# Attention, channel mixing and an eight-expert MoE on one core: who makes the experts' low weight parts, and where the routing steps stand in the queues

## The reference, cut to what matters

```python
logits = x @ w_gate                       # 8 experts
local_gate = sigmoid(x @ w_local)
for s in range(S):                        # per batch row
    fresh_e = argmax(logits[b, s])
    e = fresh_e if s == 0 or local_gate[b, s] < 0.5 else prev_e
    prev_e = e
    p = softmax(logits[b, s])
    h = maximum(x[b, s] @ w1[e], 0)       # 512 -> 1024
    out[b, s] = p[e] * (h @ w2[e])        # 1024 -> 512
```

## Time and profile before

| | us |
|---|---|
| median of 3 runs | 630.22 (628.58 to 631.71) |
| the profiled execution, whole time | 632.64 |
| its span in the trace | 630.8 |
| TensorE busy | 611.1 (97% of the span) |
| VectorE busy | 421.8 (67%) |
| ScalarE busy | 321.1 (51%) |
| GpSimd busy | 176.6 (28%) |

### The profile page before, as it was taken

How to read it: one execution, slowest core, us unless ns; L and a number is a source line. 1 busy time by engine, 2 the same in 40 slices (tenths; PEclk the granted TensorE clock), 3 DMA queues, 4 the chain that set the end, 5 groups by cost and what they waited for, 6 DMA issues and landing times.

```text
span 630.8 us, 14748 instructions
## 1 busy us (share of the span) xinstructions
PE 611.1 (97%) x4474; PEld 506.3 (80%) x4475; DVE 421.8 (67%) x1167; ACT 321.1 (51%) x698; POOL 176.6 (28%) x261
## 2 busy tenths in 40 slices
PE   8989999999999999999999899689999999999996
PEld 6878888888888888889889777568878888878885
DVE  4767779755788797686889958863772633683541
ACT  5766779687426605713527553343851612662531
POOL 4545445600000000000000600535572351184141
PEclk9999999999999999999999999979999999999999
DMA  8987886002200010010024552477792441385000
GB/s 312 372 264 244 275 276 200 18 4 81 100 35 0 1 68 0 0 47 22 0 96 179 177 217 68 131 233 236 226 330 92 156 174 48 118 308 212 20 17 15
DMA packets 32935, 84.66 MB, mean 134 GB/s; under 512 B 4602, under 2 KB 7418, under 8 KB 32896
## 3 DMA queue, kind: packets, MB, share of 16 engines
q1 hardware_dynamic: 26816, 70.03, 32.4%
q0 software_dynamic: 3200, 8.92, 4.1%
q10 hardware_dynamic: 2880, 5.24, 2.5%
HBM read 76.04 MB, written 9.70 MB: 136 GB/s over the span
## 4 chain that ended last, share of the span: by engine, by line
PE 94%; DVE 2%; issue 2%; ACT 1%; POOL 0%; DVEq 0%; ACTq 0%; POOLq 0%
PE banks L891 24%; PE banks L893 23%; PE banks L892 23%; PE banks L762 4%; PE banks L829 3%; PE banks L1081 3%; PE banks L838 2%; PE banks L792 2%; PE banks L776 2%; PE banks L806 1%; PE banks L802 1%; PE banks L1000 1%; PE banks L853 1%; DVE we_lo L1535 1%; DVE table L1755 1%
## 5 line engine op out<-in xcount | busy, mean ns | idle before, releaser
L1502 DVE CUSTOM_DVE_ANT_0 product<-x,xT 128x512 f32<-128x512 f32 x120 | 77.6, 686 | 1.4 <-DMA xT<-in_w 1.4
L891 PE MATMUL banks<-we_hi,xg_hi 128*128 (+1 forms) x160 | 66.2, 413 | 9.9 <-DVE we_lo L1535 8.0
L1799 ACT ACTIVATE prob<-neg,negmax 128x160 f32<-128x160 f32 (+1 forms) x136 | 59.1, 436 | 30.5 <-DVE negmax L1210 20.8
L1777 DVE TENSOR_SCALAR hid<-banks 128x512 f32<-128x512 f32 x34 | 23.5, 691 | 72.0 <-PE banks L893 70.8
L891 PE MATMUL banks<-we_hi,hid_hi 128*128 (+1 forms) x160 | 67.2, 420 | 0.3 <-DVE hid_lo L1616 0.2
L1909 ACT ACTIVATE k_sum<-banks 128x512 f32<-128x512 f32 (+2 forms) x40 | 21.4, 534 | 88.4 <-PE banks L893 84.8
L651 POOL TENSOR_TENSOR we_lo<-raw_end,we_hi 128x512 f32 (+1 forms) x36 | 54.6, 1545 | 35.4 <-ACT we_hi L1889 35.3
L893 PE MATMUL banks<-we_hi,xg_lo 128*128 (+1 forms) x160 | 63.8, 399 | 0.0
L892 PE MATMUL banks<-we_lo,xg_hi 128*128 (+1 forms) x160 | 63.6, 398 | 0.0
L893 PE MATMUL banks<-we_hi,hid_lo 128*128 (+1 forms) x160 | 62.7, 392 | 0.0
L892 PE MATMUL banks<-we_lo,hid_hi 128*128 (+1 forms) x160 | 62.6, 391 | 0.0
(11 more groups left out here) (298 smaller groups left out, 1465.9 us busy)
## 6 DMA issues: line engine op xcount, KB each, us to landing
xT<-in_w_e SPq DMA_DIRECT2D x36, 512.0 KB, 4.5
raw_end<-in_w_e SPq DMA_DIRECT2D x36, 512.0 KB, 5.3
qk<-in_qk_t SPq DMA_DIRECT2D x32, 448.0 KB, 6.3
vw<-in_v_t SPq DMA_DIRECT2D x32, 256.0 KB, 5.5
w_raw<-in_w_mix ACTq DMA_DIRECT2D x20, 256.0 KB, 4.3
x_rows<-x SPq DMA_DIRECT2D x17, 256.0 KB, 2.0
xT<-in_w SPq DMA_DIRECT2D x8, 256.0 KB, 3.6
vz<-in_v_z SPq DMA_DIRECT2D x8, 128.0 KB, 3.4
```

The costliest lines, as they stand in the source:

```text
L891: pe.matmul(dst, left[0], right[0], start=first, stop=False)
L1502: dve.tensor_tensor_reduce(product[:, k % 2, :], x2[:, t, :], w9(e), 1.0, 0.0, ALU.mult, ALU.add, dot[:, t % 2, e:e + 1]).then_inc(dotted, 1)
L1777: dve.tensor_scalar(hid[:, D * h:D * (h + 1)], ps_h[:, h, :], 0.0, None, ALU.max).then_inc(hid_ready, 1)
L1799: act.activation(prob[:, t % 2, c], neg[:, c], ACT.Exp, scale=-1.0, bias=negmax[:, t % 2, k:k + 1], accum_out=rsum[:, t % 2, k:k + 1]).the ...
```

## The change

GpSimd waits, before the first expert's parts 6 and 7, until VectorE has made all six of its own. For the second expert, GpSimd makes none: VectorE makes the parts 4 to 7 in a row, and GpSimd only waits for them before it scatters tile 2. The computation of `table` moves ahead of `rest_of_hidden(2, 0)`, behind the one-hot matrices of the gates. On VectorE `rest_of_hidden(0, 0)` now comes before `fresh_choice(final)` and `rest_of_hidden(0, 1)` before the logit differences and `runs`. On TensorE `turn_keeps`, `turn_last_runs` and `turn_carries` move one or two steps of `outputs(0)` later, and `turn_chosen` and `count_picks` move into `hidden(1)`, whose steps are `c`.

```diff
@@ GpSimd
             gather(2, 0, NA * P)
+            pool.wait_ge(we_lo_ready, VPARTS + VPARTS)
             last_parts(0, slice(0, 1))
@@ GpSimd, after scatter(0) and scatter(1)
-            last_parts(1, slice(1, 2))
+            pool.wait_ge(we_last_lo_ready, 3 * LPARTS)
             pool.wait_ge(y_stored[0], 16)
             scatter(2, 0)
@@ TensorE
             outputs(0, 0, first, range(0, 1))
-            turn_keeps(final)
             turn_hidden(0, 1)
             outputs(0, 0, first, range(1, 3))
+            turn_keeps(final)
+            outputs(0, 0, first, range(3, 5))
             turn_last_runs(final)
-            outputs(0, 0, first, range(3, 5))
+            outputs(0, 0, first, range(5, 7))
             turn_carries(final)
-            outputs(0, 0, first, range(5, 7))
-            turn_chosen(final)
             outputs(0, 0, first, range(7, FC)).then_inc(y_summed, 1)
...
             hidden(1, first, 0, range(0, 1))
+            turn_chosen(final)
+            hidden(1, first, 0, range(1, 3))
             count_picks(final)
-            hidden(1, first, 0, range(1, DC)).then_inc(hid_summed, 1)
+            hidden(1, first, 0, range(3, DC)).then_inc(hid_summed, 1)
@@ VectorE
+            rest_of_hidden(0, 0)
             fresh_choice(final)
-            rest_of_hidden(0, 0)
+            rest_of_hidden(0, 1)
             dve.tensor_tensor(ldiff[:], logit[:, :, 0:E], by_token(lmax[:], E), ALU.subtract).then_inc(diff_ready, 1)
             runs(final)
-            rest_of_hidden(0, 1)
             carries(final)
...
             ins.then_inc(gate_onehots_ready, 1)
-            rest_of_hidden(2, 0)
-            rest_of_part(1, slice(1, 2), 2)
-            dve.wait_ge(gates_summed, 1)
...
-            rest_of_part(1, slice(1, 2), 3)
-            rest_of_hidden(2, 1)
-            rest_of_rows(3)
+            end = ntile[0:1, 1, :].unsqueeze(1).broadcast_to([1, LATER, E])
...
+            dve.tensor_copy(table[:, MT + EARLY:2 * MT], differs).then_inc(tables_ready, 1)
+            rest_of_hidden(2, 0)
+            rest_of_part(1, slice(1, 2), 2)
+            dve.wait_ge(gates_summed, 1)
...
+            rest_of_part(1, slice(1, 2), 3)
+            rest_of_hidden(2, 1)
+            rest_of_rows(3)
-            for j in range(PARTS // 2, VPARTS):
+            for j in range(PARTS // 2, PARTS):
                 rest_of_part(1, slice(1, 2), j)
```

More of the change, by code:

```diff
@@ L1727, in _ @@
             ins.then_inc(gate_onehots_ready, 1)
-            rest_of_hidden(2, 0)
-            rest_of_part(1, slice(1, 2), 2)
-            dve.wait_ge(gates_summed, 1)
-            dve.tensor_reduce(slot_gate[:, 0:EARLY], ps_chain_odd[:, 0:3 * EARLY].rearrange("p (k m) -> p m k", k=3), AX.X, ALU.add)
-            dve.tensor_reduce(slot_gate[:, EARLY:MT], ps_chain[:, 0:3 * LATER].rearrange("p (k m) -> p m k", k=3), AX.X,
-                              ALU.add).then_inc(gates_ready, 1)
-            rest_of_part(1, slice(1, 2), 3)
-            rest_of_hidden(2, 1)
-            rest_of_rows(3)
             end = ntile[0:1, 1, :].unsqueeze(1).broadcast_to([1, LATER, E])
@@ L1755, in _ @@
             dve.tensor_copy(table[:, MT + EARLY:2 * MT], differs).then_inc(tables_ready, 1)
-            for j in range(PARTS // 2, VPARTS):
+            rest_of_hidden(2, 0)
+            rest_of_part(1, slice(1, 2), 2)
+            dve.wait_ge(gates_summed, 1)
+            dve.tensor_reduce(slot_gate[:, 0:EARLY], ps_chain_odd[:, 0:3 * EARLY].rearrange("p (k m) -> p m k", k=3), AX.X, ALU.add)
+            dve.tensor_reduce(slot_gate[:, EARLY:MT], ps_chain[:, 0:3 * LATER].rearrange("p (k m) -> p m k", k=3), AX.X,
+                              ALU.add).then_inc(gates_ready, 1)
+            rest_of_part(1, slice(1, 2), 3)
+            rest_of_hidden(2, 1)
+            rest_of_rows(3)
+            for j in range(PARTS // 2, PARTS):
                 rest_of_part(1, slice(1, 2), j)
```

## The result

The changed kernel takes 620.71 us (median of 6 runs, 618.67 to 621.44) against 631.44 for the kernel before in its 6 runs: a ratio of 0.9831, 95% interval 0.9805 to 0.9857. That is 10.7 us less (9.0 to 12.3 by the interval), where 12.0 were forecast (618.2 against the 630.22 that was known then, a ratio of 0.981). The forecast median itself was 2.5 us too low; 1.2 of that is the median of the kernel before, which was 630.22 in the three runs known then and is 631.44 in six. The profiled execution took 620.91 (forecast 620.6), with a span of 619.0 against 630.8.

What follows compares the result with a forecast made beforehand. TensorE, 94% of the span, was taken to bound the kernel, so only its idle or slow-clock time counts. 3.4 - 0.6 + 9.15 + 0 = 11.95, say 12.0 us: 630.2 to 618.2 us, range 616.2 to 622.4.

Steps and rivals of the forecast that it cites:

- Step 1, the first gap: TensorE before the first expert: GpSimd's wait removes 1.9 us idle and 1.5 us of slow clock, 3.4 us won.
- The 1.5 us of slow clock: TensorE's 3.2 us behind the gap at the first expert, at granted clock 0.53: 1.5 us lost there, to be won.
- Step 2, the choice chain: Routing turns and counts behind more matmuls: TensorE stalls 0.6 us after `count_picks`, before `outputs(1)`; bounds 0 and 1.5.
- Step 3, the tables: TensorE at the loop's first tile: 7.55 us idle less 0.4 left open, plus 2.0 of slow clock, 9.15 us won.
- the entry's 2.5 us: Register and branch work between the table read and the loop's first matmul; all but 0.4 us hidden (bounds 0 and 2.5).
- Step 4, the parts on VectorE: Second expert's parts 6 and 7 on VectorE: 0 us on the path, four parts ending 0.6 us before needed.
- the bound of 4.7: GpSimd's row copy for scatter 1 can be held up to 4.7 us by VectorE's four parts; 0 on the path.
- The open entry: Rival at the loop's first tile: 2.5 us stay instead of 0.4 and the clock falls, 622.3 us; chance 0.13.
- a chain with several stalls: Rival in the routing steps: the choice chain stalls TensorE at more steps and the clock falls, 620.6 us; chance 0.09.
- that GpSimd was not the cause: Rival for both large TensorE gaps: they stay and only the 0.6 us stall is felt, 630.8 us; chance 0.03.
- The slower case: Rival: GpSimd's scatters hold VectorE's four parts, 23.6 us instead of 4.7, 18.3 on TensorE: 636.5 us; chance 0.03.
- the kind of VectorE instruction that the prediction names: VectorE instruction with both inputs in SBUF, said to contend with GpSimd instructions reading SBUF; one with a PSUM input doesn't.

Runs made afterwards that it cites:

- the tables alone: Kernel before with only the block that makes `table` moved up ahead of `rest_of_hidden(2, 0)`: 623.13 us, ratio 0.9881.
- the parts alone: Kernel before with only the second expert's parts 6 and 7 moved from GpSimd to VectorE: 623.33 us, ratio 0.988.
- the wait alone: Kernel before with only GpSimd's wait added before the first expert's parts 6 and 7: 629.11 us, ratio 0.9963.
- the old order behind the new wait: Changed kernel with the routing steps on TensorE and VectorE put back in their old order: 620.92 us, ratio 0.9843.
- the kernel with tables and drains: Kernel before with `table` moved up and a drain after each GpSimd subtraction of the first two experts; GpSimd keeps its parts: 626.75 us, ratio 0.9916.
- the drains: Kernel before with a GpSimd drain after each of its four subtractions for the first and the second expert: 624.08 us, run one time.
- the tiny multiplication: Kernel before with four unused 128x4 VectorE multiplications ahead of VectorE's parts 2 and 3 of the first expert: 631.34 us, run one time.

## Why the prediction was right, point by point

**Step 1, the first gap.** The idle 1.9 us went, through GpSimd's place as forecast: the pair took 2.35 us, GpSimd's four stood at 361.73 to 366.77 (forecast 361.8 to 366.9), the first matmul followed without a gap. The 1.5 us of slow clock is the term that is least sure. It was in the profile before, but in the three other profiles with the same gap (1.91, 1.92 and 2.22 us) the clock stayed at 1.00. The whole executions say the same: the two kernels that keep this gap alone (the tables alone and the parts alone) have a mean granted clock of 0.997 to 1.000 in their eight runs, the changed kernel 0.996 to 1.000 in its eleven. One fall in four would give about 0.4 us on the mean, an estimate from so few; 11.5 less 1.1 is 10.4, and 10.7 was measured. The kernel with the wait alone points the other way: it gained 2.1 us (1.3 to 3.5), where the gap less the new stall of 1.22 is 0.7, the full 1.5 of clock makes it 2.2, and even 1.3 asks for 0.6 of it. So the size of this term stays open between 0 and 1.5 us, and the interval of the whole (9.0 to 12.3) holds all of that.

**Step 2, the choice chain.** Forecast 0.6 us of stall before `outputs(1)`, found 0.70. Its cause was as laid out: with `count_picks` one step earlier the stall is gone. None of the other steps stalled. What I did not cost was the other side of the move: the old order behind the new wait has a stall of 1.22 us, because `fresh_choice` is held. So behind the wait the new order gains 0.5 us by the profiles.

**Step 3, the tables.** The cast took 0.17 us and there is no gap at the loop, where I left 0.4 open. That the entry's 2.5 us is otherwise open is shown by the kernel with the parts alone: 2.19 us. So it is the early `tables_ready` that hides it under queued matmuls. The rest of the entry came up on another engine: ScalarE stands until 403.05 for a store, does its register work then, and starts rounding at 405.80. The prediction weighed the entry for TensorE alone and left ScalarE's out; `hid_lo` came 0.76 us too late. Two paths lead there from the late rounding and end together. VectorE's `rest_of_hidden(3, 0)` is queued behind a part that needs the rounding; that part ends at 408.33. And it needs ScalarE's `round_hidden`, which is queued behind two roundings of weights and ends at 408.29:

```profile
407.71 0.58 ACT L1964 ACTIVATE hid_hi<-banks 128x512 fp32r<-128x512 f32 x1
```

The kernel with ScalarE's read moved shows that ScalarE's late start was the cause; which of the two paths counts it doesn't tell, as both moved with it. This stall is the one term that the prediction's sum lacks. That the entry, put at 0.4 us for TensorE, cost nothing there makes up half of it, and that is luck.

**Step 4, the parts on VectorE.** No cost, as forecast: 4.62 us for four, over at 404.50, and the ReLU behind them waits for TensorE (0.40 us). GpSimd's row copy was held at 400.11 for 1.04 us, below the bound of 4.7. I credited the move with nothing. Alone it wins as much as the tables alone (0.988 each), because either of them ends the meeting of cast and subtractions. The forecast for the whole is not touched by this, since the credit was given to the tables. Together they don't add: the second one takes the stall from 1.6 to 0.8 us or the open entry to nothing, and frees GpSimd's queue for its gathers; the kernel with tables and drains shows what late gathers can cost (a gap of 4.31 us).

**The rivals.** The open entry is refuted for TensorE; a chain with several stalls is refuted; that GpSimd was not the cause is refuted by the drains, which leave all work and all orders as they were and only keep the four subtractions apart. The slower case, VectorE's four parts held by the scatters, did not come: 4.62 us with two DMA issues beside them.

**What stays open.** When a held VectorE instruction is let in. In three places (the pair, the cast, the tiny multiplication) it met the start of GpSimd's run and was held over all four subtractions; with the wait alone it came during the third and was let in before the fourth. No run here tells what decides. The order of the starts alone doesn't: the cast of the kernel before has its start at 404.68, inside a DMA issue of GpSimd and 0.56 us ahead of the first subtraction (405.24), and was held all the same, while in the kernel with the parts alone, where no subtraction follows the issue, it wasn't.

```profile
404.21 1.00 POOL L683 DMA_INDIRECT out_rows<-y,rows_out  x1 [0.92 <-POOL rows_out L679]
```

The cast also reads one tile in SBUF and not two, so the kind of VectorE instruction that the prediction names is not all that is held; `lmax`, with one input too, took its usual 0.30 us beside GpSimd's subtractions. It is not shown either what GpSimd waits for in the 3.8 to 4.1 us behind a drain.

## What to carry to other kernels

A long time on a trivial instruction (5.5 us for 24 numbers) is a wait in disguise: look at what the other engine of the pair does in exactly that stretch, and compare the ends. Where two engines block each other, move the run of one to where the other is idle or reads PSUM, and see what is queued behind both. Two edits that each remove the same meeting don't add; cost them as alternatives, and the second by what it does besides.

## What the runs showed of the hardware that I had not expected

A VectorE instruction of 128x4 numbers with both inputs in SBUF was held 4.84 us by a run of four GpSimd subtractions. The Trainium skill ("SBUF — State Buffer", Who interferes with whom) has the loser wait until the first instruction finishes; by that it would have been 1.2. The two steps held in the kernel with the wait alone agree with it (0.80 and 1.46 us, each let in as one subtraction ended), the pair, the cast and the tiny multiplication don't. A drain between the subtractions brought the hold down to that size (1.0 us for the pair). It had a price that no run explains: 0.2 to 0.7 us of idle GpSimd behind some drains, but 3.8 to 4.1 behind the first one in three of the four rows of subtractions that had drains.

The clock did not always follow a gap: 1.90 us of idle TensorE was followed by 0.53 in one execution, and four gaps of 1.91 to 2.22 us by 1.00 in three others. Gaps of 3.91, 4.31 and 7.55 us were followed by 0.63, 0.50 and 0.54 in the windows read here.
